# A 128-partition transform in one product for both tables, with its sums split by other engines

## The chip, the cores and the metric

The kernel runs on one core of one Trainium2 chip. The metric is the device time of one execution in microseconds. Three runs of the kernel before gave 1248.34, 1249.17 and 1250.05 us; the median is 1249.17 us.

## The reference

The input x has 4 batches of 4224 positions with 192 channels. Three layers follow each other.

```python
# 1: a causal convolution of 7 taps along the positions, softmax weights, one set per head
# 2: u = x + V-U mixing along the positions;  out = u + max(u @ w1a, 0) @ w2a
x = moe(attn(x))
# 3:
X = np.fft.fft(np.fft.fft(x, axis=1), axis=2)
u = x + np.real(X)
un = (u - mean(u)) / sqrt(var(u) + 1e-6)
out = u + np.maximum(un @ w_ch1, 0) @ w_ch2
```

The change touches only the Fourier transform along the 4224 positions of layer 3.

## The kernel before, in words

All products run in fp32r, which keeps fewer bits than f32. Each f32 operand is therefore held as a high part (the value copied to fp32r) and a low part (the value less its high part), and a product is made of high x high, high x low and low x high.

**Blocks and slots.** The work is 88 blocks of 384 positions, 11 per batch and phase. Phase 0 is layers 1 and 2, phase 1 is layer 3. Their order is phase 0 of batch 0 (blocks 0 to 10), phase 0 of batch 1 (11 to 21), phase 1 of batch 0 (22 to 32), phase 0 of batch 2 (33 to 43), phase 1 of batch 1 (44 to 54), phase 0 of batch 3 (55 to 65), then phase 1 of batches 2 and 3 (66 to 87). A block has six slots, written (block, m) with m from 0 to 5. In a slot TensorE does `up_slot` (L781; the first product of the channel layer, for the slot two ahead; it starts at L787), then the slot's extra work, then `down_slot` (L797, the second product). ScalarE's `hidden` (L992) makes the high part of what `up_slot` gave, VectorE's `lows` (L1193) the low part. The end of a block is `partial` on ScalarE (L1002), `add_residual` on VectorE (L1199) and `add_partial` on GpSimd (L1448).

**The transform.** 4224 is 128 x 33. The part along 128 is called a transform here: 11 per batch, numbered u = 0 to 10, 44 in all. Its input is `xf` (128 x 576), a sum or difference of two blocks of positions (`fold_sum`, `fold_difference`, L1238, L1252). ScalarE's `x2_high` (L1013) makes `x2h` from it, VectorE's `x2_low` (L1256) makes `x2l`, and TensorE's `dft128` (L855) multiplies both with the table `f1t` (high and low). It works on three tiles of 132 columns; the first 128 channels go to one PSUM bank, the last 64 to the other, three products per tile and half. `spectrum_high` (L1030) on ScalarE and `spectrum_low` (L1260) on VectorE then write the high and low parts of the result to `zh`, `zl` (128 channels) and `zs` (64 channels, both parts). When all 11 are there, 22 groups (`group_in`, `group_out`) do the part along 33 and the channels.

**What sets the order.** Each engine runs its instructions in one order, written out as a loop over the slots, in which dictionaries such as `dft_at` and `made_at` (L309 to L326) say which extra work stands in which slot. The six short pieces of work that go through PSUM (low rank, turn, convolution, part of t, transform, groups) share two banks, `tb`, in the order of `fill` (L374). A piece starts on TensorE when its bank was freed (`empty`) and ends with VectorE's increment of `tb_free`. In phase 0 a transform is usually at (block, 4), its `x2h` and `x2l` are made in slot 2. At the end of each batch's phase 0, two transforms stand close together: for batches 1 to 3 at slots 0 and 4 of the next block (blocks 22, 44, 66), for batch 0 at slots 3 and 5 of block 11. Of batch 1 the first seven are put off, since `zh` still holds batch 0: their `x2h` and `x2l` are stored to HBM and fetched again in blocks 21 to 25.

Of the kernel before, what the change touches and what calls it, by code (L numbers as in the profile page):

```python
# [6 lines left out]
F32 = mybir.dt.float32  # L7
# [45 lines left out]
PUT_OFF = 7  # L53
# [93 lines left out]
def program(nc, x, weight, U, V, w1a, w2a, w1b, w2b, f1, low, high, bc, mirror, backward_in, ident_in, out):  # L147
# [7 lines left out]
    x2s = hbm("x_two_split", (PUT_OFF, 2, 128, TB, D))  # L155
# [3 lines left out]
    with ExitStack() as ctx:  # L159
# [78 lines left out]
        back = sb("back", [128, NB // 2 + 1], I32)  # L238
        vlate = sb("vlate", [4 * R, (V_PARTS[2][1] - V_PARTS[2][0]) * 128], F32R)
# [69 lines left out]
        made_at, made_low_at, dft_at, put_at = {}, {}, {}, {}  # L309
        later = [NB + u for u in range(PUT_OFF)]  # L310
        for b in range(B):
            n0 = at[(0, b, 0)]
            for u in range(NB):
                w = b * NB + u
                last_two = (0, 4) if b else (3, 5)
                spot = (n0 + u + 2, 4) if u < NB - 2 else (n0 + NB, last_two[u - NB + 2])
                made = (n0 + NB - 1, 5) if u == NB - 2 else (spot[0], spot[1] - 2)
                low_made = made
                made_at[made], made_low_at[low_made] = w, w
                if w in later:  # L320
                    put_at[(made[0], made[1] + 2)] = w
                else:
                    dft_at[spot] = w
        for w, spot in zip(later, ((10, 0), (12, 0), (12, 4), (13, 0), (13, 4), (14, 0), (14, 4))):
            dft_at[(at[(0, 1, 0)] + spot[0], spot[1])] = w
        dft_order = [dft_at[spot] for spot in sorted(dft_at)]  # L326


        held = sorted([(spot, w, "made") for spot, w in made_at.items()] +
                      [(spot, w, "fetched") for spot, w in dft_at.items() if w in later])  # L330
        ahead_of = {held[k][1:]: held[k - 1][1:] for k in range(1, len(held))}
        fetch_at = {((n - 1, 5) if m == 0 else (n, 1)): w for (n, m), w in dft_at.items() if w in later}
# [13 lines left out]
        for c in range(1, B):  # L346
            n0, n1 = at[(0, c - 1, 0)], at[(0, c - 1, 0)] + NB
            if c == 2:
                spots = [(n0, 1), (n0 + 9, 1), (n0 + 10, 1), (n1, 1), (n1 + 1, 1), (n1 + 1, 3), (n1 + 2, 3), (n1 + 3, 1)]
                stores = [(n0 + 9, 3), (n1, 3), (n1 + 1, 5), (n1 + 3, 3)]  # L350
                loads = [(n0 - NB + 7, 1), (n0 - NB + 9, 1), (n0 + 10, 1), (n1 + 1, 1)]
                parts = [(n0 + 9, 5), (n1, 5), (n1 + 2, 1), (n1 + 3, 5)]
                t_last[(n1 + 4, 3)] = c
# [34 lines left out]
        for n in range(LAST + 1):  # L388
            nx = following(n)
            for m in range(M6):  # L390
                if m == 0 and nx is not None and phase(nx) == 0:
                    fill_both("low", nx, False)
# [6 lines left out]
                if (n, m) in t_part:  # L399
                    fill(("t",) + t_part[(n, m)], 0, False)  # L400
# [9 lines left out]
         act_x2h, dve_x2l, x2_out, x2_in, mix_in,  # L410
# [5 lines left out]
            "act_x2h dve_x2l x2_out x2_in mix_in "  # L416
# [5 lines left out]
        f1_in = [sem(f"f1_in{n}") for n in range(2)]  # L422
        u_in = [sem(f"u_in{n}") for n in range(UR)]
# [99 lines left out]

        def spectrum_rows(z, w):

            u = w % NB
            pairs = z[:, :, :, 1:N2].rearrange("p n k (r j) -> p n r k j", r=2)
            if u < NB - 1:
                return [pairs[:, u % 2, :, :, u // 2 * TB:u // 2 * TB + TB]]
            return [z[:, :, :, 0], pairs[:, :, :, :, HALF - 1]]  # L530

        def spectrum_parts(o, w):

            tiles = o[:, 0:TB * 2 * KC].rearrange("p (t r k) -> p t r k", t=TB, r=2)
# [13 lines left out]
        def _(e):  # L548
# [47 lines left out]
            def load_f1(k):  # L596
                if k >= 2:
                    full(e, ("dft", dft_order[k - 2], 1))
# [5 lines left out]
            def put_off(n):  # L604
                k = later.index(n)
                e.wait_ge(dve_x2l, n + 1)
                e.dma_start(x2s[k, 0], x2h[:].bitcast(F32)).then_inc(x2_out, 16)
                e.dma_start(x2s[k, 1], x2l[:].bitcast(F32)).then_inc(x2_out, 16)

            def fetch(n):  # L610
                k = later.index(n)
                e.wait_ge(x2_out, (k + 1) * 32)
                x2_free(e, n, "fetched")
                e.dma_start(x2h[:].bitcast(F32), x2s[k, 0]).then_inc(x2_in, 16)
                e.dma_start(x2l[:].bitcast(F32), x2s[k, 1]).then_inc(x2_in, 16)
# [106 lines left out]
            for n in range(LAST + 1):  # L722
                nx, pv = following(n), previous(n)
                for m in range(M6):
# [41 lines left out]
                    if done in dft_at:  # L766
                        k = dft_order.index(dft_at[done]) + 2
# [12 lines left out]
        def _(e):  # L780
# [74 lines left out]
            def dft128(n):  # L855
                k = dft_order.index(n)
# [707 lines left out]
```

## Time and profile before

| | us |
|---|---|
| median of three runs | 1249.17 |
| the profiled execution, its own time | 1250.71 |
| its span, first to last instruction | 1248.9 |
| busy: TensorE, VectorE, ScalarE, GpSimd | 1217.2, 829.3, 678.6, 425.5 |

The busy time of an engine is the union of its instructions' times. A product's end is modelled and reaches over the start of the next, so a busy TensorE can still be waiting by some tenths of a microsecond. The better measure is the distance from one start to the next. In this document an `up_slot` begins with an L787, so the distance of two neighbouring L787 is the length of a slot. The span is the execution's time less 1.8 us. The profiled execution was 1.54 us slower than the median of the three runs.

### The profile page before, as it was taken

To read this page: it belongs to the slowest core of one execution; us is meant where nothing else is said; L and a number is where in the kernel's file an instruction comes from. 1 tells how busy PE (TensorE), PEld (TensorE's weight loads), DVE (VectorE), ACT (ScalarE), POOL (GpSimd) and SP (SyncE) were. 2 spreads that over 40 slices of the span, in tenths; PEclk is the share of its full clock that TensorE was granted. 3 is DMA by queue.
4 is the path that set the end of the run, shared out by engine and by line. 5 is a ranking of instruction groups with operands and counts; after the bars stand their busy time and mean duration, and the time that the engine had idled before them with its cause. 6 is when DMAs were issued, how large, how long until landed. Compare 5 with 4: busy or idle time off the path is not lost.

```text
span 1248.9 us, 23838 instructions
## 1 busy us (share of the span) xinstructions
PE 1217.2 (97%) x8404; PEld 1189.6 (95%) x8404; DVE 829.3 (66%) x2235; ACT 678.6 (54%) x1779; POOL 425.5 (34%) x542
## 2 busy tenths in 40 slices
PE   6799999999999999999999999999999999999998
PEld 5799999999998999999999999999999999999998
DVE  5565576777775577655556877755666777766654
ACT  5355555444566655445555665544445656565554
POOL 0133342343343244323333344421212344533331
PEclk9899999999999999999999999999999999999999
DMA  8867543344556533224434322222323233222220
GB/s 291 278 202 227 178 142 91 105 134 136 162 180 215 184 119 93 75 69 133 130 103 139 115 91 89 93 63 79 98 93 106 77 109 92 92 94 86 86 68 30
DMA packets 87680, 154.48 MB, mean 124 GB/s; under 512 B 11449, under 2 KB 46628, under 8 KB 87517
## 3 DMA queue, kind: packets, MB, share of 16 engines
q1 hardware_dynamic: 79944, 133.95, 34.0%
q0 software_dynamic: 7616, 18.99, 4.7%
q8 instruction: 68, 1.11, 0.4%
q14 instruction: 52, 0.42, 0.1%
HBM read 94.59 MB, written 63.32 MB: 126 GB/s over the span
## 4 chain that ended last, share of the span: by engine, by line
PE 91%; SPq 2%; DMA 2%; DVE 2%; issue 1%; POOL 1%; ACT 1%; POOLq 0%; ACTq 0%
PE bank L806 20%; PE bank L807 9%; PE bank L787 8%; PE bank L794 7%; PE bank L795 7%; PE bank L791 7%; PE bank L788 7%; PE bank L810 4%; PE bank L905 3%; PE bank L840 2%; PE bank L868 2%; PE bank L928 2%; PE bank L870 2%; PE bank L869 2%; PE bank L809 2%; PE bank L889 1%
## 5 line engine op out<-in xcount | busy, mean ns | idle before, releaser
L1000 ACT ACTIVATE ht<-bank 128x384 fp32r<-128x384 f32 x528 | 259.0, 491 | 472.1 <-PE bank L795 468.1
L1196 DVE SCALAR_TENSOR_TENSOR ht<-bank,ht 128x384 fp32r<-128x384 f32 x528 | 293.6, 556 | 332.7 <-ACT ht L1000 322.6
L806 PE MATMUL bank<-w,ht 128*128 128x384 f32 x1320 | 418.7, 366 | 0.8 <-DVE ub L1204 0.5
L807 PE MATMUL bank<-w,ht 128*128 128x192 f32 x1320 | 331.0, 251 | 0.0
L1450 POOL TENSOR_TENSOR ub<-ub,tmp 128x576 f32<-128x576 f32 x88 | 125.8, 1430 | 459.4 <-DVE ub L1204 310.7
L806 PEld LDWEIGHTS bank<-w,ht 128*128 128x128 f32 x1320 | 248.9, 189 | 3.9 <-issue 3.1
L807 PEld LDWEIGHTS bank<-w,ht 128*128 128x128 f32 x1320 | 252.4, 191 | 0.0
L787 PE MATMUL bank<-uth,w1h 128*128 128x384 f32 x528 | 189.4, 359 | 0.0
L794 PE MATMUL bank<-uts,w1s 128*128 128x384 f32 x528 | 179.0, 339 | 0.6 <-DVE uts L1229 0.6
L791 PE MATMUL bank<-utl,w1h 128*128 128x384 f32 x528 | 178.8, 339 | 0.5 <-DVE utl L1221 0.5
L788 PE MATMUL bank<-uth,w1l 128*128 128x384 f32 x528 | 178.7, 338 | 0.0
L795 PE MATMUL bank<-uts,w1t 128*128 128x384 f32 x528 | 178.2, 337 | 0.0
L1499 POOL DMA_INDIRECT mixed<-rowm,mir x84 | 82.7, 985 | 217.3 <-DVE rowm L1302 214.3
L788 PEld LDWEIGHTS bank<-uth,w1l 128*128 128x128 f32 x528 | 101.3, 192 | 0.0
L794 PEld LDWEIGHTS bank<-uts,w1s 128*128 128x128 f32 x528 | 99.4, 188 | 1.8 <-DVE uts L1229 1.5
L791 PEld LDWEIGHTS bank<-utl,w1h 128*128 128x128 f32 x528 | 99.7, 189 | 1.2 <-DVE utl L1221 1.2
L787 PEld LDWEIGHTS bank<-uth,w1h 128*128 128x128 f32 x528 | 100.1, 190 | 0.5 <-issue 0.5
L795 PEld LDWEIGHTS bank<-uts,w1t 128*128 128x128 f32 x528 | 99.5, 188 | 0.0
L810 PE MATMUL bank<-w,ht 128*128 128x384 f32 x264 | 81.9, 360 | 0.0
L1473 POOL TENSOR_TENSOR xhl<-xin,xhl 128x432 fp32r<-128x432 f32 (+1 forms) x48 | 52.5, 1116 | 82.8 <-ACT xhl L990 82.8
L809 PE MATMUL bank<-w,ht 128*128 128x192 f32 x264 | 66.7, 253 | 0.0
L868 PE MATMUL bank<-f1t,x2h 128*64 128x132 f32 (+1 forms) x264 | 62.6, 250 | 4.0 <-issue 3.4
(125 smaller groups left out, 2271.4 us busy)
## 6 DMA issues: line engine op xcount, KB each, us to landing
f1t<-f_copy SPq DMA_DIRECT2D x44, 396.0 KB
ub<-x_two SPq DMA_DIRECT2D x44, 288.0 KB
mix<-mixed SPq DMA_DIRECT2D x44, 288.0 KB, 3.3
out<-ub SPq DMA_DIRECT2D x44, 288.0 KB
xin<-in_x SPq DMA_DIRECT2D x12, 864.0 KB, 6.2
x_conv<-xin SPq DMA_DIRECT2D x12, 756.0 KB
vch<-v_split SPq DMA_DIRECT2D x42, 192.0 KB
mixed<-rowk SPq DMA_DIRECT2D x88, 74.2 KB
```

Source lines behind the costliest of these rows:

```text
L787: e.matmul(o, w1h[ph][:, c], uth[:, par], start=True, stop=False)
L788: e.matmul(o, w1l[ph][:, c], uth[:, par], start=False, stop=False)
L791: e.matmul(o, w1h[ph][:, c], utl[:, par], start=False, stop=False)
L794: e.matmul(o, w1s[ph][:, c], uts[:, par], start=False, stop=False)
L795: e.matmul(o, w1t[ph][:, c], uts[:, par], start=False, stop=True).then_inc(pe_up, 1)
L806: e.matmul(dn[t][:, 0:2 * D], hh, w2[ph][:, m, :], start=(m == 0), stop=False)
L807: mm = e.matmul(dn[t][:, 0:D], hl, w2[ph][:, m, 0:D], start=False, stop=False)
L809: e.matmul(dn[t][:, 0:D], hl, w2[ph][:, m, 0:D], start=False, stop=False)
L810: e.matmul(dn[t][:, 0:2 * D], hh, w2[ph][:, m, :], start=False, stop=True)\
L1000: e.activation(hth[q % 4], up[q % 3][:, 0:TOK], ACT.Relu).then_inc(act_h, 1)
L1196: e.scalar_tensor_tensor(htl[q % 4], up[q % 3][:, 0:TOK], 0.0, hth[q % 4].bitcast(F32), ALU.max, ALU.subtract).then_inc(dve_l, 1)
L1450: e.tensor_tensor(u_slot(n), u_slot(n), tmp[:], ALU.add).then_inc(pool_y, 1)
```

## The change

- Each of a transform's three tiles now has a step of its own, `dft_tile`. It multiplies the high part of the first 128 channels with the high and low tables in one product of 264 columns, where there were two of 132. The 64 other channels keep three products of 132 columns; they go to the same bank. A tile has 5 products, a transform 15, where it had 18.
- The two halves of 132 columns must then be added. ScalarE copies the first to a new buffer `zt`, VectorE adds the second to it (`tile_sum`). When three tiles are in `zt`, ScalarE makes `zh` from it (`spectrum_high`) and GpSimd `zl` (`spectrum_low`). `zs` is made tile by tile from PSUM by ScalarE and VectorE.
- Tiles 0 and 1 stand in the transform's slot, tile 2 in a later one. Usually (block, 4) and (block, 5); the split of `zt` is two slots after that, or in the third tile's own slot for transforms 8, 9 and 10 and for the put-off ones.
- The ends of the batches' phase 0 are laid out anew (see `made`, `spot`, `third` in the diff): for batches 1 to 3 transforms 9 and 10 are at slots 0 and 3, their third tiles at 1 and 4, and what transform 10 needs is made in slot 1. For batch 0 they are at slots 1 and 4.
- Six transforms are put off, not seven, and `xf` is stored and fetched in place of `x2h` and `x2l`; they stand at slots 0 and 3 of blocks 23 to 25. The convolution of batch 2 moves to other slots, and parts of t use the other bank.

```diff
             for u in range(NB):
                 w = b * NB + u
-                last_two = (0, 4) if b else (3, 5)
-                spot = (n0 + u + 2, 4) if u < NB - 2 else (n0 + NB, last_two[u - NB + 2])
-                made = (n0 + NB - 1, 5) if u == NB - 2 else (spot[0], spot[1] - 2)
...
                 if w in later:
-                    put_at[(made[0], made[1] + 2)] = w
+                    put_at[slot_after(*fold_at[w], 2)] = w
+                    spot = (n1 + 1 + u // 2, u % 2 * 3)
+                    made, third = slot_after(*spot, -1 if u % 2 == 0 else -2), slot_after(*spot, 1)
+                elif u < NB - 2:
+                    made, spot, third = [(n0 + u + 2, m) for m in (2, 4, 5)]
+                elif u == NB - 2:
+                    made, spot, third = (n1 - 1, 5), (n1, 0 if b else 1), (n1, 1 if b else 3)
+                else:
+                    made, spot, third = [(n1, m) for m in ((1, 3, 4) if b else (3, 4, 5))]
+                made_at[made], dft_at[spot], third_at[third] = w, w, w
+                split = slot_after(*third, 2) if w not in later and u < NB - 3 else third
...
-                spots = [(n0, 1), (n0 + 9, 1), (n0 + 10, 1), (n1, 1), (n1 + 1, 1), (n1 + 1, 3), (n1 + 2, 3), (n1 + 3, 1)]
+                spots = [(n0 + 9, 1), (n0 + 9, 3), (n0 + 10, 0), (n0 + 10, 3), (n1, 5), (n1 + 1, 5), (n1 + 2, 5), (n1 + 3, 5)]
...
+        def x2_free(e, w):
+            k = dft_order.index(w)
+            if k:
+                full(e, ("dft", dft_order[k - 1], 2))
...
+            def dft_tile(w, t):
...
+                bk, q = empty(e, ("dft", w, t))
+                xh, xl, wave, both = x2h[:, t], x2l[:, t], f1t[:, k % 2, 0, t, :], f1t[:, k % 2, :, t, :]
+                e.matmul(bk[:, 0:4 * KC].rearrange("p (a c) -> p a c", a=2), xh[:, 0:128], both, start=True, stop=False,
+                         skip_group_check=True)
+                e.matmul(bk[:, 0:2 * KC], xl[:, 0:128], wave, start=False, stop=True, skip_group_check=True)
+                o = bk[0:64, 4 * KC:6 * KC]
+                e.matmul(o, xh[:, 128:D], wave, start=True, stop=False, skip_group_check=True)
+                e.matmul(o, xh[:, 128:D], both[:, 1], start=False, stop=False, skip_group_check=True)
+                e.matmul(o, xl[:, 128:D], wave, start=False, stop=True, skip_group_check=True).then_inc(pe_tb[q], 1)
...
                 if g == 0:
-                    taken(e, ("dft", n_, 0))
                     taken(e, ("dft", n_, 1))
+                    taken(e, ("dft", n_, 2))
+                    e.wait_ge(pool_zl, (b + 1) * NB)
...
+            def tile_out(w, t):
+                if t == 0:
+                    wait(e, pool_zl, dft_order.index(w))
...
+                o, q = full(e, ("dft", w, t))
+                copy(zt[:, t * 2 * KC:(t + 1) * 2 * KC], o[:, 0:2 * KC])
+                copy(spectrum_row(zs[0:64], w, t), spectrum_part(o[0:64], 2)).then_inc(act_tb[q], 1)
+
+            def spectrum_high(w):
+                k = dft_order.index(w)
+                e.wait_ge(dve_zt, (k + 1) * TB)
+                for rows, part in zip(spectrum_rows(zh[:], w), spectrum_sums(w)):
+                    last = copy(rows, part)
+                last.then_inc(act_zh, 1)
...
+            def tile_sum(w, t):
+                o, q = copied(e, ("dft", w, t))
+                row = zt[:, t * 2 * KC:(t + 1) * 2 * KC]
+                e.tensor_tensor(row, o[:, 2 * KC:4 * KC], row, ALU.add).then_inc(dve_zt, 1)
+                e.tensor_tensor(spectrum_row(zs[64:128], w, t), spectrum_part(o[0:64], 2),
+                                spectrum_row(zs[0:64], w, t).bitcast(F32), ALU.subtract).then_inc(tb_free[q], 1)
...
+            def spectrum_low(w):
+                e.wait_ge(act_zh, dft_order.index(w) + 1)
+                for low, part, high in zip(spectrum_rows(zl[:], w), spectrum_sums(w), spectrum_rows(zh[:], w)):
+                    last = e.tensor_tensor(low, part, high.bitcast(F32), ALU.subtract)
+                last.then_inc(pool_zl, 1)
```

On TensorE, ScalarE and VectorE the third tile's step stands right after `up_slot`, `hidden` or `lows` of its slot. On ScalarE `spectrum_high` stands after `turned_high` and before the two `tile_out` and `x2_high` of the slot. On VectorE `x2_low` stands last in its slot, after `fold_sum` and `statistics` of slot 1.

## Rows read from the trace of the kernel before

**Rows 1.** Page: busy time by engine; the chain that ended last.

```profile
PE 1217.2 (97%) x8404; PEld 1189.6 (95%) x8404; DVE 829.3 (66%) x2235; ACT 678.6 (54%) x1779; POOL 425.5 (34%) x542
...
PE 91%; SPq 2%; DMA 2%; DVE 2%; issue 1%; POOL 1%; ACT 1%; POOLq 0%; ACTq 0%
```

**Rows 2.** Timeline, TensorE, a transform (start us, us, engine, line, operation); lines left out.

```profile
570.78 0.30 PE L868 MATMUL bank<-f1t,x2h 128*128 128x132 f32 x1
...
571.82 0.23 PE L868 MATMUL bank<-f1t,x2h 128*64 128x132 f32 x1
...
572.37 0.39 PE L806 MATMUL bank<-w,ht 128*128 128x384 f32 x1
...
572.69 0.36 PE L806 MATMUL bank<-w,ht 128*128 128x384 f32 x1
...
572.98 0.36 PE L806 MATMUL bank<-w,ht 128*128 128x384 f32 x1
```

**Rows 3.** Timeline, TensorE: where slots begin (L787), and one wait.

```profile
688.83 0.36 PE L787 MATMUL bank<-uth,w1h 128*128 128x384 f32 x1
...
693.70 0.36 PE L787 MATMUL bank<-uth,w1h 128*128 128x384 f32 x1
...
695.46 0.34 PE L787 MATMUL bank<-uth,w1h 128*128 128x384 f32 x1
...
696.15 0.34 PE L795 MATMUL bank<-uts,w1t 128*128 128x384 f32 x1
...
696.76 0.30 PE L868 MATMUL bank<-f1t,x2h 128*128 128x132 f32 x1 [0.27 <-issue]
...
699.23 0.36 PE L787 MATMUL bank<-uth,w1h 128*128 128x384 f32 x1
...
870.05 0.36 PE L787 MATMUL bank<-uth,w1h 128*128 128x384 f32 x1
...
873.35 0.36 PE L787 MATMUL bank<-uth,w1h 128*128 128x384 f32 x1
```

**Rows 4.** Timeline, ScalarE and VectorE, around 695 us.

```profile
694.80 0.49 ACT L1000 ACTIVATE ht<-bank 128x384 fp32r<-128x384 f32 x1 [0.52 <-PE bank L795]
695.19 0.68 ACT L990 ACTIVATE x2h<-xf 128x576 fp32r<-128x576 f32 x1
...
695.90 0.76 DVE L1258 TENSOR_TENSOR x2l<-xf,x2h 128x576 fp32r<-128x576 f32 x1
```

**Rows 5.** Groups of instructions by form, ScalarE (busy us, mean ns of one).

```profile
L1000 ACT ACTIVATE ht<-bank 128x384 fp32r<-128x384 f32 x528 | 259.0, 491 | 472.1 <-PE bank L795 468.1 <-issue 1.6 <-PE bank L807 1.4
...
L990 ACT ACTIVATE x2h<-xf 128x576 fp32r<-128x576 f32 x44 | 29.9, 679 | 0.4
...
L990 ACT ACTIVATE qb<-bank 99x98 f32<-99x98 f32 x88 | 21.8, 247 | 2.2 <-PE bank L939 2.1
...
L990 ACT ACTIVATE zs<-bank 64x396 fp32r<-64x396 f32 x40 | 23.7, 594 | 0.4 <-PE bank L870 0.4
...
L990 ACT ACTIVATE zs<-bank 64x132 fp32r<-64x132 f32 x4 | 1.9, 467 | 0.0
```

**Rows 6.** Groups by form, VectorE.

```profile
L1258 DVE TENSOR_TENSOR x2l<-xf,x2h 128x576 fp32r<-128x576 f32 x44 | 34.8, 792 | 1.3
...
L1301 DVE TENSOR_TENSOR rowk<-bank,qb 99x97 f32<-99x97 f32 x88 | 21.7, 246 | 1.0 <-ACT qb L990 1.0
...
L1264 DVE TENSOR_TENSOR zs<-bank,zs 64x132 fp32r<-64x132 f32 x4 | 1.6, 400 | 0.1
```

**Rows 7.** Groups by form, GpSimd.

```profile
L1473 POOL TENSOR_TENSOR xhl<-xin,xhl 128x384 fp32r<-128x384 f32 x12 | 12.2, 1038 | 25.4 <-ACT xhl L990 25.4
```

**Rows 8.** Timeline, VectorE and GpSimd, where the two meet.

```profile
685.19 2.25 DVE L1250 TENSOR_TENSOR xf<-ub 128x576 f32<-128x576 f32 x1
...
685.37 1.44 POOL L1455 TENSOR_TENSOR ub<-ub,mix 128x576 f32<-128x576 f32 x1
```

**Rows 9.** Windows, 380.8 to 436.2 us (busy time of each engine, clock, DMA).

```profile
380.80:436.20 55.40, 53.08 (x371) 51.01 (x370) 29.63 (x75) 33.63 (x86) 19.70 (x29) 0.97 0.64 208
```

More of the change, by code:

```diff
@@ L51 @@
 HALF = N2 // 2
-PUT_OFF = 7
+PUT_OFF = 6
 ROWS = 3
@@ L326, in program @@
+                made_at[made], dft_at[spot], third_at[third] = w, w, w
+                split = slot_after(*third, 2) if w not in later and u < NB - 3 else third
+                split_at[split], split_low_at[slot_after(*split, 1) if split != third else split] = w, w
         dft_order = [dft_at[spot] for spot in sorted(dft_at)]
-        held = sorted([(spot, w, "made") for spot, w in made_at.items()] +
-                      [(spot, w, "fetched") for spot, w in dft_at.items() if w in later])
-        ahead_of = {held[k][1:]: held[k - 1][1:] for k in range(1, len(held))}
@@ L332, in program @@
-        fetch_at = {((n - 1, 5) if m == 0 else (n, 1)): w for (n, m), w in dft_at.items() if w in later}
+        assert dft_order == [third_at[spot] for spot in sorted(third_at)] == [made_at[spot] for spot in sorted(made_at)]
+        made_of = {w: spot for spot, w in made_at.items()}
+        xf_before = {}
+        for half in range(2):
+            held = [(spot, w, "folded") for w, spot in fold_at.items() if w % NB % 2 == half]
+            for w in later[half::2]:
+                ahead_ = max((made_of[v], v) for v in fold_at if v % NB % 2 == half and made_of[v] < made_of[w])
+                fetch_at[slot_after(*ahead_[0], 1)] = w
+                held.append((slot_after(*ahead_[0], 1), w, "fetched"))
+            held.sort()
+            for k in range(1, len(held)):
+                xf_before[held[k][1:]] = held[k - 1][1:]
@@ L422, in program @@
         f1_in = [sem(f"f1_in{n}") for n in range(2)]
+        x2_out = [sem(f"x2_out{n}") for n in range(2)]
+        x2_in = [sem(f"x2_in{n}") for n in range(2)]
         u_in = [sem(f"u_in{n}") for n in range(UR)]
@@ L602, in load_f1, with put_off, fetch @@
                 e.dma_start(f1t[:, k % 2].bitcast(F32), f1d[:, i]).then_inc(f1_in[k % 2], 16)
[L604 to L615, printed above, removed]
+            def put_off(w):
+                e.wait_ge(dve_xf, w + 1)
+                e.dma_start(x2s[later.index(w)], xf[:, w % NB % 2]).then_inc(x2_out[w % NB % 2], 16)
+            def fetch(w):
+                e.wait_ge(x2_out[w % NB % 2], (later.index(w) // 2 + 1) * 16)
+                xf_free(e, w, "fetched")
+                e.dma_start(xf[:, w % NB % 2], x2s[later.index(w)]).then_inc(x2_in[w % NB % 2], 16)
             def load_x(c, p):
@@ L981, in _ @@
                     if (n, m) in dft_at:
-                        dft128(dft_at[(n, m)])
+                        for t in range(2):
+                            dft_tile(dft_at[(n, m)], t)
                     down_slot(n, m)
@@ L1013, in x2_high @@
             def x2_high(w):
-                e.wait_ge(dve_xf, w + 1)
-                x2_free(e, w, "made")
+                if w in later:
+                    e.wait_ge(x2_in[w % NB % 2], (later.index(w) // 2 + 1) * 16)
+                else:
+                    e.wait_ge(dve_xf, w + 1)
+                x2_free(e, w)
                 copy(x2h[:], xf[:, w % NB % 2]).then_inc(act_x2h, 1)
@@ L1171, in _ @@
                         turned_high(nx)
+                    if (n, m) in split_at:
+                        spectrum_high(split_at[(n, m)])
                     if (n, m) in dft_at:
-                        spectrum_high(dft_at[(n, m)])
+                        for t in range(2):
+                            tile_out(dft_at[(n, m)], t)
                     if (n, m) in made_at:
@@ L1230, in turned_low @@
                                     ALU.subtract).then_inc(tb_free[q], 1)
-            def xf_free(w):
-                before = max([v for v in range(w) if v % NB % 2 == w % NB % 2], default=-1)
-                wait(e, act_x2h, before + 1)
-                wait(e, dve_x2l, before + 1)
             def fold_sum(n):
@@ L1434, in _ @@
                     if (n, m) in dft_at:
-                        spectrum_low(dft_at[(n, m)])
-                    if (n, m) in made_low_at:
-                        x2_low(made_low_at[(n, m)])
+                        for t in range(2):
+                            tile_sum(dft_at[(n, m)], t)
+                    if (n, m) in made_at:
+                        x2_low(made_at[(n, m)])
                     if (n, m) in t_last:
```

121 lines of the change are left out of this document (58 added, 63 removed).

## The prediction

> **What bounds the kernel now.** I read the page first. TensorE is busy 97% of the span and is 91% of the chain that ended last [rows 1]; VectorE (66%) and ScalarE (54%) have room on average. Next I read TensorE's timeline for distances of starts, since a product's modelled end hides short waits. A transform's slot with nothing late takes 873.35 - 870.05 = 3.30 us [rows 3], so TensorE is the bound nearly everywhere, and what it executes is paid in full. Longer slots show where something else ends last. Slot (44,0) takes 699.23 - 695.46 = 3.77 us and slot (43,4) 693.70 - 688.83 = 4.87 us [rows 3], both where a batch's phase 0 ends. The change gives where TensorE is the bound (44 transforms) and takes where other engines are (the four ends of phase 0, and blocks 23 to 25).
>
> **TensorE's products.** Nine products with 128 columns of weights take 571.82 - 570.78 = 1.04 us, the first a little more than the others: 0.113 each. Nine with 64 columns take 572.37 - 571.82 = 0.55: 0.060 each [rows 2]. Both move 132 columns, so the weight load sets the first kind. With 384 columns a product takes (696.15 - 695.46) / 4 = 0.173 [rows 3], 0.45 ns per column; there the columns set it. A pair of 384 and 192 columns takes 572.98 - 572.69 = 0.29 [rows 2], which is 0.173 and 0.117 for the shorter one, more than its columns need (0.086): the next load of 128 columns sets it. So a product costs the longer of its own columns and the next weight load.
> - Before: 9 products before a 128-column load (the last is followed by L806's) at 0.113, and 9 at 0.060: 1.557 us.
> - After, per tile: 264 columns x 0.45 = 0.119; three followed by 64-column loads, 0.180; the last, followed by a 128-column load, 0.113: 0.412. Three tiles: 1.236.
> - 0.321 us x 44 = 14.1 us less. Bounds: nothing (if only columns counted), and 14.1.
>
> The Trainium skill, "TensorE: Matmul & The Clock Gate" (LDWEIGHTS), gives a load as its columns divided by 1.2 GHz, 107 ns for 128; the trace agrees with its 113.
>
> **ScalarE, VectorE, GpSimd per transform.** The trace has no contiguous copy of 132 columns. ScalarE takes 0.247 for 98 and 0.491 for 384 [rows 5], so I estimate 0.28 by a line between them. A strided one of 132 takes 0.467 [rows 5]. A `tile_out` is then 0.75, and about 0.67 since neighbours overlap (in rows 4 `x2h` starts 0.39 after a `hidden` of 0.49). Before, ScalarE had two copies of about 0.594; after, 3 x 0.67 and one of 0.59: 2.6 against 1.2. VectorE: the sum of 132 is near 0.246 for 97 columns, I take 0.29, and `zs` 0.400 [rows 6], 2.1 for three tiles against two of about 0.58. GpSimd gets a new operation of 396 elements, by that of 384 at least 1.04 [rows 7]; it writes strided, which no row shows on GpSimd, so up to twice that.
>
> **In usual places** (about 30 transforms) this is hidden. Counted from the start of (block,4), TensorE ends tile 0 at 1.3 and tile 1 at 1.7, and the third tile asks for bank 0 at 3.5. ScalarE has copied tile 0 by 2.2, VectorE freed the bank by 2.9. The third tile's bank is asked for again by the low rank product 0.87 after the block ends; VectorE frees it 0.6 after the end. `add_residual` ends 0.25 later than now, with 0.3 to spare. I cost this at 0; if the cover of 0.2 to 0.3 is gone, 0.1 x 30 = 3 us. `x2h` and `x2l` stay two slots ahead.
>
> **Transform 9, made in slot 5.** Now, around 695 us: `hidden` ends at 695.29, `x2h` at 695.87, `x2l` at 696.66 [rows 4] and the product starts at 696.76, where TensorE could have at 696.33, which is 0.87 after the slot's start [rows 3]: 0.43 waited. After, ScalarE's slot 5 has, between `hidden` and `x2_high`: `tile_out` of transform 8's third tile (0.67), the wait for VectorE's sum (0.3), and `spectrum_high` (0.6). That is 1.6 more before `x2h` starts; TensorE comes 0.41 later by the third tile. Net 1.2 more, in blocks 22, 44 and 66. In block 22 the convolution's high parts stand in (21,4), so the queue there is longer: 1.7. (There is also a new wait of 0.4 for bank 0 at (21,5), and one of 0.55 in (21,4) goes; I set them against each other.) In block 11 no product waits for it, but `add_residual` stands behind `x2_low` on VectorE, and `down_slot` waits for that: 1.25 more. Sum: 1.25 x 3 + 1.7 = 5.4.
>
> **Transform 10, made in slot 1.** `x2_high` waits for `fold_sum`, which on VectorE now stands behind `tile_sum`; on ScalarE `hidden` and `turned_high` of slot 2 queue behind `x2_high`, and `x2_low` comes behind `statistics`. Counted from the start of slot 1: `fold_sum` ends 3.9, `x2h` 4.6, `hidden` 5.1, `turned_high` 6.2, `x2l` 5.6, `lows` 6.1, the turn's banks are free at 7.1 and 7.8. TensorE asks for them at 5.3 and tile 1 ends at 8.3, not 6.2: 2.1 waited, where 0.37 was in slot 4. That is 1.75 in blocks 44 and 66. In block 22, TensorE runs a part of t in slot 1, which covers it: 0. In block 11 it is a chain like transform 9's, 1.6 against 0.4: 1.2. Sum: 4.7.
>
> **Other terms at the ends.** `group_in` of slot 0 now waits for GpSimd's last `zl`, and `down_slot` for a later `add_residual`: 0.7 in batches 2 and 3, 0.4 in batch 1, -0.25 in block 12: 1.5. Slot (43,4) and its like in batch 3: the chain from `add_residual` is 0.25 later and `x2l` 0.15: 0.8 together. Blocks 23 to 25 take 55.4 us now, of which TensorE is busy 53.1 and ScalarE 33.6 [rows 9]. By my ledger of slots a block with two transforms and a convolution takes 17.5 there with 15.0 of products, since each `x2h` of slot 5 follows two convolution copies; that is 6.5 to 7 of waits in three blocks against 4.6 now: 2.1, with bounds of -3 and 5. Fewer put-off transfers (12 for 28) remove a late fetch at block 24, which is in this number. Sum of the paragraph: 4.4.
>
> **The shared path.** A `fold_sum` that met GpSimd's add ran 2.25 us, until shortly after GpSimd's own 1.44 and the next small operation [rows 8]. `zl` starts on GpSimd just before `x2_low` at the ends, and can hold it for up to 0.6, at eight places. I take 2 us, bounds 0 and 5.
> The Trainium skill, "SBUF — State Buffer" (Who interferes with whom), says that VectorE with two SBUF inputs and a reading GpSimd exclude each other for whole instructions; the trace agrees, with that 2.25. The rule speaks against this change.
>
> **The sum.** 5.4 + 4.7 + 4.4 + 2 = 16.5 more, 14.1 less: 2.4 more. On the profiled execution's 1250.71 that is 1253.1. It was 1.54 above the median, so the median becomes 1251.6.
>
> **Rivals.**
> - *The saving comes through.* The queues at the ends recover sooner than in my ledger, which adds whole durations; only transform 9's 1.2 and half of the rest stay, 5.4 + 5.5 = 11 at most and 4 at least: 1239 to 1246, middle 1243. For it: ScalarE and VectorE are idle a third of the time [rows 1]. Against: the chains at 695 us leave no room already [rows 4].
> - *ScalarE and VectorE set the pace in blocks 20 to 25* (slower, decided in slot 5 and slot 0 of blocks 22 to 25). Per block ScalarE has about 15.8 of work for 15.0 of products. If each of the eight transforms there waits 1.5 and not 0.8, and `zl` takes 2 and not 1, that is 5.5 and 3 more: 1260. Against: rows 9 show ScalarE at 61% there.
> - *A product costs its columns alone.* Both versions stream 2376 columns, so TensorE saves nothing and the ends cost 16.5: 1266. Rows 2 speak against it: 132 columns take 0.113 or 0.060 by their weights. The Trainium skill, "TensorE: Matmul & The Clock Gate" (Back-to-back issue gap), gives columns / 2.4 + 2.5 ns; that is 57 ns here, right for 64 columns of weights (60) and wrong for 128 (113).
>
> **How the numbers follow.** A difference of 0.2% (2.5 us) is about what can be told from none. The forecast case, the two terms nearly cancelling, has 0.55 and its own range 1247 to 1257; 0.25 of it lies within 0.2%, 0.30 above. The first rival has 0.29 (0.25 faster, 0.04 within), the second 0.12, the third 0.04. So faster 0.25, same 0.29, slower 0.46. The range 1243 to 1259 leaves out the lower part of the first rival (0.10), half of the second (0.06) and the third (0.04).
>
> **What would show it.** TensorE: usual slots 4 and 5 together 4.8 us where they were 5.05, transform products 54 us in all for 68. ScalarE's busy time up by about 60 us, VectorE's by 40, GpSimd's by 45 or more. Slot (44,0) with a wait of 1.7 before its first tile, slot (44,3) with 2, and `x2l` longer where `zl` runs. It is wrong if usual slots have waits (then slower), if the waits in blocks 11, 22, 44 and 66 stay as they are (then near 1241), or if a tile takes over 0.5 us.

## The result, and the profile after

| | before | after |
|---|---|---|
| median of four runs on one chip, us | 1248.78 | 1282.97 |
| lowest and highest | 1248.34, 1250.05 | 1279.63, 1285.65 |
| ratio to before, 95% interval | | 1.0277, 1.026 to 1.0293 |
| the profiled execution, its span | 1250.71, 1248.9 | 1281.67, 1279.8 |
| mean granted clock, share of full | 0.993 | 0.988 |

The changed kernel is 2.8% slower. The forecast was 1251.6 us, with a range up to 1259. The two profiled executions, from which the places below are read, lie 31.0 us apart, the medians 34.2.

The page of the changed kernel, busy time and the chain that ended last, answers to [rows 1]:

```profile
PE 1215.5 (95%) x8272; PEld 1180.8 (92%) x8272; DVE 883.1 (69%) x2403; ACT 714.9 (56%) x1995; POOL 486.2 (38%) x590
...
PE 85%; DVE 5%; issue 3%; DMA 2%; ACT 2%; POOL 2%; SPq 1%; POOLq 0%; ACTq 0%
```

TensorE fell from 91% of the chain to 85%, VectorE rose from 2 to 5%. Groups by form, all engines, after (answers to [rows 5 to 7]):

```profile
L1514 POOL TENSOR_TENSOR zl<-zt,zh 128x396 fp32r<-128x396 f32 x40 | 57.1, 1428 | 82.3 <-ACT zh L1032 82.2
L1309 DVE TENSOR_TENSOR x2l<-xf,x2h 128x576 fp32r<-128x576 f32 x44 | 53.7, 1221 | 8.6 <-ACT x2h L1032 7.7
L1032 ACT ACTIVATE zs<-bank 64x132 fp32r<-64x132 f32 x132 | 53.5, 406 | 0.0
...
L1032 ACT ACTIVATE zt<-bank 128x132 f32<-128x132 f32 x132 | 38.8, 294 | 29.4 <-PE bank L909 28.2
L1314 DVE TENSOR_TENSOR zt<-bank,zt 128x132 f32<-128x132 f32 x132 | 38.6, 292 | 11.5 <-ACT zs L1032 9.3
```

The row to look at is one that nobody changed: `x2l`, the same operation as before, takes 1221 ns on average where it took 792 [rows 6].

Distances of `up_slot` starts (L828 after, L787 before) add up over regions as follows. "Forecast" is the prediction's sum set out by place: 0.32 less per transform, its terms for the ends, and 1.5 for the pair of convolution pieces that moves from block 11 to block 20.

| blocks | forecast, us | measured, us |
|---|---|---|
| 0 to 10 (nine usual transforms) | -2.9 | +12.0 |
| 11 to (12,0) | +0.1 | +3.4 |
| 19 to 34 (end of batch 1, put-off ones) | +2.2 | +6.6 |
| 35 to 42 (eight usual) | -2.6 | +1.4 |
| 43 to (45,0) | +3.1 | +5.0 |
| 57 to 64 (eight usual) | -2.6 | -2.0 |
| 65 to (67,0) | +3.1 | +5.3 |
| shared path, in no place | +2.0 | |
| all | +2.4 | +31.4 |

The miss is 29.0 us. Half of it is in the first row, of which blocks 7 to 9 alone have +11.0. Timeline of the changed kernel in block 7, all engines, lines left out:

```profile
152.37 1.39 POOL L1514 TENSOR_TENSOR zl<-zt,zh 128x396 fp32r<-128x396 f32 x1 [3.11 <-ACT zh L1032]
...
153.90 0.98 POOL L1548 DMA_INDIRECT ub<-x_conv,back  x1
...
154.90 2.01 POOL L1533 TENSOR_TENSOR xhl<-xin,xhl 128x384 fp32r<-128x384 f32 x2
...
155.88 3.41 DVE L1309 TENSOR_TENSOR x2l<-xf,x2h 128x576 fp32r<-128x576 f32 x1
...
156.88 1.79 POOL L1565 TENSOR_TENSOR w1l<-w1l_raw,w1h 128x768 fp32r<-128x768 f32 x1
...
159.39 0.36 PE L903 MATMUL bank<-f1t,x2h 128*128 128x264 f32 x1 [2.33 <-issue]
...
161.21 0.58 PE L828 MATMUL bank<-uth,w1h 128*128 128x384 f32 x1
...
163.41 0.31 PE L909 MATMUL bank<-f1t,x2l 128*64 128x132 f32 x1
```

And the kernel before at the same place:

```profile
148.75 0.97 POOL L1488 DMA_INDIRECT ub<-x_conv,back  x1 [0.16 <-issue]
...
153.30 2.04 POOL L1473 TENSOR_TENSOR xhl<-xin,xhl 128x384 fp32r<-128x384 f32 x2 [3.57 <-ACT xhl L990]
...
155.22 0.76 DVE L1258 TENSOR_TENSOR x2l<-xf,x2h 128x576 fp32r<-128x576 f32 x1
...
155.28 2.39 POOL L1505 TENSOR_TENSOR w1l<-w1l_raw,w1h 128x768 fp32r<-128x768 f32 x1
...
156.23 0.22 PE L868 MATMUL bank<-f1t,x2h 128*128 128x132 f32 x1
```

Before, `x2l` started when the convolution's low parts (`xhl`) were all but through, and 0.06 us ahead of GpSimd's `w1l`. (`w1l` is the first of three long operations, one in each of blocks 7, 8 and 9, that make the low parts of layer 3's weights.) `x2l` took 0.76, and `w1l` 2.39. After, `zl` stands in slot 2 of GpSimd's order, ahead of the indirect load in slot 3, and waits for `zh` until 152.37. So the load starts at 153.90 and not at 148.75, and `xhl` starts 0.95 us later, counted from the block's start (146.81, before 146.16). `x2l` is issued 9.07 after the block's start, as before, but now in the middle of `xhl`, which `w1l` follows without a gap. `x2l` takes 3.41 and ends (159.29) 0.62 after `w1l` (158.67), which takes only 1.79. The two engines changed roles, and TensorE waits 2.33. Blocks 3, 5, 36 and 38 show the same with one GpSimd operation less: 1.82 to 1.91. In blocks 57 to 64, where no convolution stands beside it, all eight are 0.76.

In block 9 `x2l` takes 0.76, and yet slot (9,4) takes 6.31 us where it took 3.38. There VectorE's two small operations that make the low part of `tst` (an operand of the V-U mixing) are caught; they too have two SBUF inputs. The changed kernel, then the kernel before:

```profile
189.08 4.16 DVE L1401 TENSOR_TENSOR tst<-tsb,tst 32x192 fp32r<-32x192 f32 x2 [0.23 <-ACT tst L1032]
```

```profile
180.55 2.02 DVE L1350 TENSOR_TENSOR tst<-tsb,tst 32x192 fp32r<-32x192 f32 x2
```

After, they start 0.20 behind the start of a `zl` (188.88) and end 0.21 behind the end (193.03) of the third weights' operation, which follows that `zl`. In x4, where neither stands there, they take 0.74 together.

The second thing to see in block 7 comes after the wait: at 161.21 an L828 takes 0.58 where others take 0.36, and at 163.41 a product of 132 columns 0.31 where others take 0.23. Windows of the changed kernel (us; busy time of PE, PEld, DVE, ACT, POOL; granted clock; DMA share; GB/s):

```profile
158.00:166.00 8.00, 6.61 (x40) 6.64 (x41) 5.73 (x13) 3.04 (x11) 0.67 (x1) 0.79 0.15 41
...
172.00:184.00 12.00, 9.66 (x58) 9.11 (x57) 9.06 (x15) 4.64 (x14) 4.72 (x4) 0.86 0.27 77
```

The same windows of the kernel before:

```profile
158.00:166.00 8.00, 8.00 (x54) 8.00 (x53) 5.02 (x11) 3.68 (x9) 3.75 (x3) 1.00 0.44 139
...
172.00:184.00 12.00, 11.91 (x79) 11.42 (x78) 10.08 (x21) 5.92 (x15) 4.07 (x2) 1.00 0.43 132
```

A clock of 0.79 is a mean: part of the window ran at 1.2 GHz, the rest at 2.4. Slot (7,5) takes 3.67 us where (9,5), the same work, takes 2.18: the low clock cost 1.5 there. It does not follow from the wait alone. The kernel of x3 (below) differs from the changed one in the ends of batches 2 and 3 only (blocks 44 and 66). In block 7 it has an `x2l` of 3.44 and a wait of 2.37, but this window:

```profile
158.00:166.00 8.00, 5.63 (x43) 5.33 (x42) 6.80 (x13) 3.42 (x12) 1.95 (x2) 1.00 0.19 55
```

Its (7,5) takes 2.17, and its blocks 7 to 9 take 49.89 us, where the changed kernel took 54.18 and the kernel before 43.16. So of the +11.0 in these blocks 6.7 came in both profiles, and 4.3 only where the clock fell.

A usual transform without such a hold, TensorE in block 58 (answers to [rows 2]):

```profile
910.48 0.36 PE L828 MATMUL bank<-uth,w1h 128*128 128x384 f32 x1
...
911.37 0.29 PE L903 MATMUL bank<-f1t,x2h 128*128 128x264 f32 x1
...
912.16 0.39 PE L847 MATMUL bank<-w,ht 128*128 128x384 f32 x1
...
915.23 0.34 PE L828 MATMUL bank<-uth,w1h 128*128 128x384 f32 x1
```

Two tiles take 912.16 - 911.37 = 0.79, and slots 4 and 5 together 915.23 - 910.48 = 4.75; before they took 5.05 in this block. The saving is there.

The end of batch 2's phase 0, slot (44,3) of the changed kernel (answers to [rows 3] and [rows 4]):

```profile
727.77 0.69 ACT L1032 ACTIVATE x2h<-xf 128x576 fp32r<-128x576 f32 x1 [0.84 <-DVE xf L1298]
...
728.32 1.39 POOL L1514 TENSOR_TENSOR zl<-zt,zh 128x396 fp32r<-128x396 f32 x1
...
728.49 1.84 DVE L1309 TENSOR_TENSOR x2l<-xf,x2h 128x576 fp32r<-128x576 f32 x1
...
731.82 0.36 PE L903 MATMUL bank<-f1t,x2h 128*128 128x264 f32 x1 [2.47 <-DVE utl L1278]
```

The slot takes 5.56 us, and (44,0) 4.78. The shapes are those of the prediction: transform 10 waits in slot 3, and `x2l` lies behind a `zl` that began 0.17 before it.
The window behind this wait, after:

```profile
732.00:740.00 8.00, 7.77 (x57) 7.33 (x57) 5.35 (x15) 6.43 (x22) 1.58 (x3) 1.00 0.18 51
```

### The profile page after: what moved, and what is told of

Its sections match the earlier page's. It is cut to its first block, busy times and chain, and to the rows that moved or that the text cites. A ratio compares the mean times of both kernels' runs of the same rounds, so it can differ in the third digit from the quotient of the medians.

```text
span 1279.8 us, 24033 instructions
## 1 busy us (share of the span) xinstructions
PE 1215.5 (95%) x8272; PEld 1180.8 (92%) x8272; DVE 883.1 (69%) x2403; ACT 714.9 (56%) x1995; POOL 486.2 (38%) x590
## 4 chain that ended last, share of the span: by engine, by line
PE 85%; DVE 5%; issue 3%; DMA 2%; ACT 2%; POOL 2%; SPq 1%; POOLq 0%; ACTq 0%
PE bank L847 19%; PE bank L848 8%; PE bank L828 7%; PE bank L835 7%; PE bank L836 7%; PE bank L832 7%; PE bank L829 7%; PE bank L851 4%; PE bank L943 4%; PE bank L881 2%; PE bank L967 2%; PE bank L903 2%; PE bank L850 2%; PE bank L927 2%; PE bank L965 1%
## 5 line engine op out<-in xcount | busy, mean ns | idle before, releaser
L828 PE MATMUL bank<-uth,w1h 128*128 128x384 f32 x528 | 189.9, 360 | 0.0
L1514 POOL TENSOR_TENSOR zl<-zt,zh 128x396 fp32r<-128x396 f32 (+2 forms) x48 | 62.7, 1311 | 113.2 <-ACT zh L1032 113.1
L828 PEld LDWEIGHTS bank<-uth,w1h 128*128 128x128 f32 x528 | 100.4, 190 | 0.6 <-issue 0.5
L903 PE MATMUL bank<-f1t,x2h 128*128 128x264 f32 x132 | 43.6, 330 | 29.4 <-issue 18.7
```

The lines of the kernel that those rows point to most:

```text
L828: e.matmul(o, w1h[ph][:, c], uth[:, par], start=True, stop=False)
```

## The experiments

Theory A: the loss in usual places is `x2l` held behind a row of GpSimd operations that `zl` delays. Theory B: it is the new work on ScalarE and VectorE, or TensorE's own products. The ends were tried apart from this. Where times of blocks or slots are given, they are of one profiled execution of each kernel.

**x1_weights_later.** The changed kernel, with `w1l` and the two operations like it moved from blocks 7 to 9 to blocks 12 to 14.

```diff
-                    if m == 4 and n in (7, 8, 9):
-                        second_low(n - 7)
+                    if m == 4 and n in (12, 13, 14):
+                        second_low(n - 12)
```

> The changed kernel with one move: GpSimd's three long operations that make the low parts of the second layer's weights (second_low) stand in blocks 12, 13, 14 instead of 7, 8, 9. Theory 1 (VectorE's x2_low, with both inputs in SBUF, is held while GpSimd works through operations that now reach it back to back, since the new zl operation delays all of them): x2_low of blocks 7 and 8 falls from 3.41 us to 0.9 to 1.9, blocks 7 to 9 together lose 10.8 us, and the time becomes about 1272. Theory 2 (blocks 7 to 9 wait because ScalarE and VectorE have more to do there): nothing moves, 1283.

Measured: 1274.40 us, ratio to before 1.0202 (1.0169 to 1.0235). Blocks 7 to 9 went from 54.18 to 43.97. Timeline, VectorE:

```profile
156.10 1.67 DVE L1309 TENSOR_TENSOR x2l<-xf,x2h 128x576 fp32r<-128x576 f32 x1
```

`x2l` still waits for the convolution's low parts, but for nothing behind them. Moving three GpSimd operations, all off the path in the kernel before, was worth 8.6 us.

**x2_zl_vector.** The changed kernel, with `spectrum_low` moved from GpSimd's loop (-) to VectorE's (+), at the same slots.

```diff
+                    if (n, m) in split_low_at:
+                        spectrum_low(split_low_at[(n, m)])
...
-                    if (n, m) in split_low_at:
-                        spectrum_low(split_low_at[(n, m)])
```

> The changed kernel with zl made by VectorE, last in the slot in which GpSimd made it. Theory 1 (the price is GpSimd's operation in the path of x2_low): the mean x2_low falls from 1.22 us to about 0.8, blocks 2 to 9 and 35 to 42 lose 11 and 3 us, the ends of the batches some 3 to 5 and VectorE's 0.6 us more costs 2 back; about 1264 (1261 to 1268). Theory 2 (ScalarE and VectorE are overloaded by the six small operations of a transform): more work for VectorE makes it slower, 1283 to 1300.

Measured: 1275.28 us, 1.0205 (1.0173 to 1.0237). Groups by form:

```profile
L1309 DVE TENSOR_TENSOR x2l<-xf,x2h 128x576 fp32r<-128x576 f32 x44 | 36.3, 824 | 8.6 <-ACT x2h L1032 7.7
...
L1321 DVE TENSOR_TENSOR zl<-zt,zh 128x396 fp32r<-128x396 f32 x40 | 30.0, 751 | 0.6 <-ACT zh L1032 0.6
```

`x2l` is back near 792, and blocks 7 to 9 take 45.41: theory A holds there. The time was missed by 11 us: `zl` now costs 0.75 of VectorE, and in blocks 23 to 25, with two transforms each, slots (24,3) and (25,3) grew from 4.41 and 4.35 to 6.59 and 6.41 us; the three blocks take 59.0 for 53.1. That is half of the miss; the other half has no single place. At the ends, slots (22,0), (44,0) and (66,0) fell by 0.7 to 0.8 (to 4.10, 4.12 and 4.09), and (44,3) did not fall (5.83).

**x6_before_plus_gpsimd.** The other direction: the kernel before, with one operation on GpSimd that nobody needs, in slot 2 after each of 25 usual transforms.

```diff
+                    if (n, m) in extra_at:
+                        some = bass.AP(ident, 0, [[128, 128], [0, 8], [1, 72]])
+                        e.tensor_tensor(zo[:].rearrange("p (a c) -> p a c", a=8), some, some, ALU.add).then_inc(zo_set, 1)
```

> The kernel before, with nothing of the change but a GpSimd operation of 576 elements (1.43 us, as long as zl) in the slot (block, 2) after each usual transform, 25 of them, started at that slot's start; its result is not used. Theory 1: x2_low is held as in the changed kernel, 3.4 us in blocks 7 and 8, 1.8 in the blocks with an indirect load in slot 3 (3, 5, 36, 38 and others): 8 to 14 us slower, 1257 to 1263. Theory 2 (the loss comes with the small operations on ScalarE and VectorE or the third tile): no change, 1249.

Measured: 1262.36 us, 1.0098 (1.0066 to 1.013). Block 7, GpSimd and VectorE:

```profile
153.41 1.15 POOL L1540 TENSOR_TENSOR zo<-ident 128x576 f32<-128x576 f32 x1 [2.87 <-PE bank L812]
...
155.70 2.00 POOL L1478 TENSOR_TENSOR xhl<-xin,xhl 128x384 fp32r<-128x384 f32 x2
...
157.16 2.94 DVE L1263 TENSOR_TENSOR x2l<-xf,x2h 128x576 fp32r<-128x576 f32 x1
```

And the window of the same kernel behind it:

```profile
160.00:168.00 8.00, 7.80 (x49) 7.84 (x50) 3.94 (x10) 3.01 (x7) 1.00 (x1) 0.79 0.18 51
```

The operation took 1.15 us and `x2l` 2.94, not the 1.43 and 3.4 of the expectation. Blocks 7 to 9 take 52.42 (43.16 before, 54.18 after), with the old products and none of the new work of ScalarE and VectorE. Even the clock of 0.79 is there, so the 12.6 us hold some of its cost: block 65, where `x2l` took 0.76 as before, is 3.8 longer, in a window (985 to 1001 us) with a mean clock of 0.79. Theory B falls for blocks 7 to 9.

**x3_ends_later.** The changed kernel; in batches 2 and 3 transform 10 is made in slot 2, stands at slots 4 and 5.

```diff
-                    made, spot, third = [(n1, m) for m in ((1, 3, 4) if b else (3, 4, 5))]
+                    made, spot, third = [(n1, m) for m in ((3, 4, 5) if b == 0 else (1, 3, 4) if b == 1 else (2, 4, 5))]
```

> The changed kernel with transform 10 of batches 2 and 3 made in slot 2 and multiplied in slots 4 and 5 (as before), not made in slot 1 and multiplied in slots 3 and 4. The wait of about 3 us at (44,3) and 2 us at (66,3) should go; group_in of slot 0 of the next block then waits for zl, which ends 2.2 us after TensorE gets there (0.4 now). Net 1 us less per batch: about 1281. If the wait at slot 3 is not from the order made in slot 1, it stays and the time rises by 3 to 4.

Measured: 1282.12 us, 1.0261 (1.0227 to 1.0294). The wait in (44,3) is gone (1.72 us, 5.56 before), but (44,4) takes 4.07 where it took 2.16 and (45,0), where `group_in` waits 1.87 for the last `zl`, 4.35 where it took 2.68. The wait moved, and nothing was won: the end of batch 2 (43 to (45,0)) takes 38.11 for 36.34, that of batch 3 36.07 for 36.60.

**x4_split_earlier.** x1 with `spectrum_high` and `spectrum_low` of usual transforms one slot earlier (the diff is against the changed kernel and leaves x1's lines out).

```diff
-                split = slot_after(*third, 2) if w not in later and u < NB - 3 else third
+                split = slot_after(*third, 1) if w not in later and u < NB - 3 else third
```

> x1_weights_later, and for the usual transforms zh and zl one slot earlier (ScalarE in slot 0, GpSimd in slot 1 of the next block, not 1 and 2), so that GpSimd is through with zl before its indirect load and the convolution's low parts. Theory 1 (x2_low is held by whatever GpSimd still has to do at its turn): x2_low falls from 1.8 to 0.9 us in blocks 3, 5, 36, 38 and from 1.66 to 0.76 in 40 and 41, slot 4 of these falls from 3.4 to 3.7 us to about 2.6 to 2.7, 5 to 6 us together: 1269. Theory 2 (an operation of GpSimd costs what it lasts wherever it stands): fold_sum in slot 1 is held instead and the time stays, 1274.

Measured: 1269.09 us, 1.0174 (1.0155 to 1.0192). Block 7, GpSimd and VectorE:

```profile
146.91 1.38 POOL L1514 TENSOR_TENSOR zl<-zt,zh 128x396 fp32r<-128x396 f32 x1
...
153.58 0.76 DVE L1309 TENSOR_TENSOR x2l<-xf,x2h 128x576 fp32r<-128x576 f32 x1
```

Blocks 2 to 9 take 118.8 us (132.5 in the changed kernel, 121.0 before), blocks 35 to 42 118.9 (122.3 and 120.9). These usual places now take 2.3 and 2.0 us less than before, nearly the 2.6 forecast for eight of them, and all that is left of the loss is at the ends and in blocks 19 to 22. (At 65 to (67,0) this profile has 3.6 more than the changed kernel's, with a mean clock of 0.72 between 1002 and 1014 us.)

**x9_high_first.** x4 with ScalarE's `x2_high` before `spectrum_high` where both are in a slot.

```diff
-                    if (n, m) in split_at:
-                        spectrum_high(split_at[(n, m)])
...
                     if (n, m) in made_at:
                         x2_high(made_at[(n, m)])
+                    if (n, m) in split_at:
+                        spectrum_high(split_at[(n, m)])
```

> x4_split_earlier, and ScalarE does x2_high before the copy zh of the same slot, where it did it after. My ledger of the ends: the wait of transform 9 at slot 0 (blocks 22, 44, 66; in block 11 add_residual) is the chain third tile, zt sum, zh, x2h, x2l; without zh and the wait for the sum in it, x2h starts 0.9 us earlier, and x2_low starts before zl and is not held (0.76 for 1.43): 1.3 to 1.5 us less in slot 0 of blocks 22, 44, 66 and 11, and about 1 in blocks 23 to 25: 5 to 8 us less than x4, 1262. If these waits come from other work (tile sums, the conv copies), no more than 2 us.

Measured: 1260.83 us, 1.0112 (1.0096 to 1.0129). Block 11, x4 and then x9, three engines:

```profile
211.77 0.66 ACT L1032 ACTIVATE zh<-zt 128x396 fp32r<-128x396 f32 x1 [0.37 <-DVE zt L1314]
...
212.32 0.67 ACT L1032 ACTIVATE x2h<-xf 128x576 fp32r<-128x576 f32 x1
...
213.03 1.43 DVE L1309 TENSOR_TENSOR x2l<-xf,x2h 128x576 fp32r<-128x576 f32 x1 [0.86 <-ACT x2h L1032]
...
214.56 0.36 PE L903 MATMUL bank<-f1t,x2h 128*128 128x264 f32 x1 [1.98 <-issue]
```

```profile
209.27 0.73 ACT L1032 ACTIVATE x2h<-xf 128x576 fp32r<-128x576 f32 x1
...
209.88 0.66 ACT L1032 ACTIVATE zh<-zt 128x396 fp32r<-128x396 f32 x1
...
210.32 0.76 DVE L1309 TENSOR_TENSOR x2l<-xf,x2h 128x576 fp32r<-128x576 f32 x1
...
211.18 0.36 PE L903 MATMUL bank<-f1t,x2h 128*128 128x264 f32 x1 [0.53 <-DVE x2l L1309]
```

`x2h` no longer stands behind the wait for `zt` and behind `zh`, and `x2l` is issued before `zl`, not behind it. Region 11 to (12,0) went from 23.3 to 18.8 us. Before it took 19.9, with the pair of convolution pieces (1.5) that has left it. Slots (22,0), (44,0) and (66,0) fell from 5.73, 4.92 and 4.79 to 3.29, 3.29 and 3.27. Later waits in the ends of batches 1 to 3 remain: (44,3) takes 5.51, where x4 had 4.26.

**x5_usual_only.** The kernel before, with the new form only for usual transforms up to u = 7, 25 in all (eight of batches 0, 2 and 3 each and, not counted in the expectation's 24, transform 7 of batch 1), and with the edits of x1 and x4; parts of t use bank 1, as in the changed kernel. All ends keep their old form.

```diff
+        tiled = [w for spot, w in sorted(dft_at.items()) if spot[1] == 4 and blocks[spot[0]][0] == 0 and w % NB <= TILED and w not in later]
```

> The kernel before, with only the 24 usual transforms (0 to 7 of batches 0, 2 and 3) in the form of the change; the others, the ends of the batches and the put-off transforms are as before. The weights' low parts and the splits stand as in x4. Theory 1 (TensorE saves 0.27 us per transform net, and the loss is GpSimd in the path of x2_low and the ends' layout): 24 x 0.27 = 6.5 us less than before, 1242 to 1244. Theory 2 (six small operations for two cost time by themselves): at or above 1249.

Measured, 10 runs beside 13: 1247.98 us for 1247.69, ratio 1.0003 (0.9991 to 1.0015). The usual blocks gave their part (2 to 9: -2.3, 35 to 42: -2.1, 57 to 64: -2.0), but blocks 43 and 65 took 1.2 more each and blocks 20 to 22 1.8 more. The expected 6.5 us did not come.

**x10_first_seven.** x5 with transform 7 in its old form too, and a part of t in bank 1 only where a third tile stands in the slot.

```diff
-TILED = 7
+TILED = 6
...
-                    fill(("t",) + t_part[(n, m)], 1, False)
+                    fill(("t",) + t_part[(n, m)], int((n, m) in third_at), False)
```

> The kernel of x5_usual_only with two edits: transform 7 of each batch keeps its old form too (21 transforms in the new form, 24 before), and a part of t uses bank 1 only in a slot that holds a third tile. Theory: what x5_usual_only lost again against its 24 gains of 0.27 us came from transform 7's third tile, which lies just before block 43 (65) and delays add_residual (blocks 43 and 65: 1.2 us each), and from t in bank 1 (blocks 20 to 22: 1.8). Then slots 43 and 65 are 14.1 again and blocks 20 to 22 50.5, and the time is 3.5 to 4 below x5_usual_only, near 1244, ratio to before 0.997. Rival: any third tile before the last usual transform of a batch delays the same chain, by one block earlier: blocks 42 and 64 take the loss, and the time stays at 1247 to 1248.

Measured: 1244.85 us (6 runs) for 1248.45 (11 runs), ratio 0.9967 (0.9955 to 0.998). 21 transforms have the new form. Slot (43,4), in x5 and then in x10 (L824 is there the first product of `up_slot`, L828 the one that needs VectorE's `utl`):

```profile
686.33 0.36 PE L824 MATMUL bank<-uth,w1h 128*128 128x384 f32 x1
...
687.95 0.44 PE L828 MATMUL bank<-utl,w1h 128*128 128x384 f32 x1 [1.09 <-DVE utl L1306]
...
692.03 0.36 PE L824 MATMUL bank<-uth,w1h 128*128 128x384 f32 x1
```

```profile
686.31 0.36 PE L824 MATMUL bank<-uth,w1h 128*128 128x384 f32 x1
...
687.10 0.44 PE L828 MATMUL bank<-utl,w1h 128*128 128x384 f32 x1 [0.26 <-DVE utl L1306]
...
691.18 0.36 PE L824 MATMUL bank<-uth,w1h 128*128 128x384 f32 x1
```

Blocks 43, 65 and 20 to 22 are back at the times of the kernel before, to 0.03 us. The rival, that the loss moves one block up, had 0.3 in block 42 and no more. The two edits were made together. In blocks 20 to 22 both apply (transform 7 of batch 1 stands in slot (20,4)), so what each gave there is not separated. This version is faster than the kernel before by 0.3%, with an interval of 0.2 to 0.45%. The weights' operations, which also stand elsewhere in it, were not moved alone in the kernel before; its blocks 7 to 9, with two transforms in the new form, are 0.6 us shorter, which those two account for.

## Why the prediction was wrong

**The step that failed** is the shared path, with the one it leaned on, "in usual places". The prediction said of `zl` that it "can hold it for up to 0.6, at eight places", 2 us with bounds of 0 and 5, and of the usual places "I cost this at 0". It looked for `zl` beside `x2_low` at the ends alone. In usual blocks both stand in slot 2, but `zl` runs first, and behind it GpSimd has a load, the convolution's low parts and, in blocks 7 to 9, the weights' operations. The new operation needed only to push these by 0.95 us (block 7) to bring them under VectorE's operations. x4 takes this away: blocks 2 to 9 fall by 13.7 and 35 to 42 by 3.4, 17 us of the 29 missed, of which 4.3 are the clock's in blocks 7 to 9. x6 puts one such operation into the kernel before, and gets 9.3 of the 11.0 in blocks 7 to 9. The prediction followed what it moved past the queues of ScalarE and VectorE, and not past GpSimd's, whose operations ended long before anyone needed them.

**The bound of the hold** was taken from one case in [rows 8], a `fold_sum` that waited for one operation. Rows above show a hold through the rest of one and a whole second one: 3.41 us, 2.65 more than undisturbed.

The Trainium skill, "SBUF — State Buffer" (Summary: rules for kernel authors), says of a VectorE operation with two SBUF inputs and a GpSimd operation that reads SBUF that the second to issue blocks until the first finishes. In block 7 before, the trace agrees: `x2l`, issued 0.06 us ahead, took 0.76, and `w1l` 2.39 for 1.79. That the second may also wait through what follows the first is only in the rows of this case.

**The clock** had no term. After the long waits of blocks 7 and 8 the granted clock was 0.79 and 0.86 in the windows shown, and (7,5) took 1.5 us more. The waits do not decide it: x3 had the same wait in block 7 at a clock of 1.00, and after the wait of 2.47 in (44,3) the changed kernel's stayed at 1.00 too. What makes the difference was not tried. Over the whole execution the mean clock fell from 0.993 to 0.988; as an estimate from these two, 1279.8 x 0.012 - 1248.9 x 0.007 = 6.6 us of the 31 are the clock's at most.

**Transforms 9 and 10 at the ends** were found in the right slots and mis-sized. Against the 2.56 that (58,4) takes with two tiles, (44,0) with 4.78 has a wait of 2.2, forecast 1.7, and (44,3) with 5.56 one of 3.0, forecast 2.1. For the three regions that end batches 0, 2 and 3 the forecast was 6.3 in all, measured 13.7. x9 shows that the order on ScalarE, `spectrum_high` before `x2_high`, was the larger part in batch 0 (4.5 us with what followed it); the prediction had 1.25 and 1.2 for the two transforms there. In slot 0 of blocks 22, 44 and 66 the same order was most of the wait: with x9's order 3.3 us are left, against 2.56. Taking `zl` from GpSimd (x2) gave 0.7 to 0.8 of it. x3 shows that a later slot only moves the wait. What makes slot 3 wait stays open. In block 44 neither x2 (5.83) nor x9 (5.51) shortened it, though `x2l` took 0.76 in both, while the profiles of x1 and x4, in the changed kernel's order there, have 4.20 and 4.26 with an `x2l` of 1.14 and 1.13. So the hold is not the whole of it, and one profile of this slot says little.

**Blocks 23 to 25** had a forecast of 2.1 more in waits, less 1.9 for six transforms and 1.5 for a convolution pair that left them: -1.3. They got 2.3 us shorter, but by slot (24,0), which held a late fetch and fell from 6.32 to 3.08; the rest of them grew by 0.9. The nearness to the forecast is luck in part: with the old layout that slot took 6.32 in x5 and 4.88 in x10. What precedes them, blocks 19 to 22, was forecast at 3.4 (waits 2.1, two convolution pairs 2.9, less five transforms' 1.6) and took 8.1 more.

**TensorE's saving** was right in kind and nearly in size: 4.75 us for slots 4 and 5 where 4.8 was forecast and 5.05 stood before. Of 0.30 there 0.05 is given back in the next slot 0 (2.09 for 2.04), in `down_slot`, whose first two products start 0.26 apart in block 59 where they started 0.19 apart; no row gives the cause. So 0.25 per usual transform arrives in blocks 57 to 64, where 0.32 was forecast.

**The durations** held: `zt` 294 ns for 280, its sum 292 for 290, `zs` 406 for 467, `zl` 1428 within 1040 to twice that. Busy time rose by 36 us on ScalarE (forecast 60), by 54 on VectorE (forecast 40; 19 of the 54 are held `x2l`), and by 61 on GpSimd (forecast 45 or more). ScalarE's is smaller because neighbouring copies overlap and busy time counts the overlap once: the durations of its transform copies add up to 123 us after and 57 before, about 66 more.

**The rivals.** That columns alone count is refuted by the 0.30. (The formula that the prediction gives there from the Trainium skill, "TensorE: Matmul & The Clock Gate" (Back-to-back issue gap), is the page's for a single product; of a stream the section says that the load and the product both set the spacing, and the 0.113 agree with that.) The rival that ScalarE and VectorE set the pace in blocks 20 to 25 had the right sign, in blocks 20 to 22 (57.4 us for 50.5, of which 2.9 are two more pairs of convolution pieces), and not the main place. The saving of the first rival is real once it is kept away from the ends and GpSimd's work is moved: x10.

## What to carry to other kernels

An engine off the critical path still times when its operations meet another engine's. Before an operation is added to GpSimd, list what follows it there without a gap, and look for each VectorE operation with two SBUF inputs that is now issued within that row; in this case its end moved to shortly after the end of the row (0.62 us in block 7, 0.21 in block 9).

A saving per instance on the bounding engine should be taken only where the chains around it have room: 21 of 44 transforms, with GpSimd's work moved out of the way, gave 3.6 us; all 44, without that, lost 34.

## What the runs showed of the hardware

- An unneeded GpSimd operation of 1.15 us, 25 times, cost the kernel 12.6 us, part of it by a lower clock, although GpSimd is busy a third of the time.
- A push of GpSimd's work by 0.95 us changed which engine waits: `x2l` 0.76 and `w1l` 2.39 where `x2l` started 0.06 ahead of `w1l` and `xhl` was all but through, 3.41 and 1.79 where `x2l` was issued in the middle of `xhl`.
- A sum with one input in PSUM (`tile_sum`) showed no such hold: 14 of the 132 ran for 0.25 us or more beside a long GpSimd operation, and none of the 132 took over 0.30.
- GpSimd's strided `zl` of 396 elements takes 1.43 us, the contiguous pair of 384 [rows 7] 1.04 each; VectorE does the strided one in 0.75.
- A wait of 2.33 us of TensorE in block 7 was followed by a window with a mean clock of 0.79; the same wait in x3 (2.37) and one of 2.47 in block 44 by windows at full clock.
